# Layer 1 as seven unrolled tiles of 288 and 384 tokens, six chunks of weights to a pair of heads, turned probabilities in the place of the loaded v

## The reference

```
q, k, v: (4, 8, 576, 64)
q_d, k_d, v_d = means over 4 neighbouring tokens           # 144 tokens
out_up    = repeat(softmax_attention(q_d, k_d, v_d), 4)
scores    = q @ k.T / 8, masked to |i - j| < 4
out_local = softmax(scores) @ v
x = (out_up + out_local) as (2304 tokens, 512)
h = x @ w_in   (512 x 2048);  g = max(0.01 h, h);  x = g @ w_out  (2048 x 512)
h = x @ w_in2  (512 x 2048);  g = h - tanh(h);     out = g @ w_out2
```

## Time and profile before

| | |
|---|---|
| median of three runs | 953.19 us |
| the profiled execution | 953.53 us |
| its span, first to last instruction | 951.8 us |
| mean granted TensorE clock | 0.998 |
| busy: TensorE, VectorE, ScalarE, GpSimd | 939.1, 541.2, 557.2, 403.1 us |
| attention of the first batch | to about 43 us |
| layer 1 with attention between its chunks | about 44 to 432 us |
| layer 1 alone | about 432 to 537 us |
| layer 2 | about 537 us to the end |

### The profile page before, as it was taken

One profiled execution on the slowest core, in us unless ns is written; L12 is line 12 of the kernel. 1 busy time (PEld: TensorE's weight loads), 2 busy tenths in 40 slices (PEclk: granted clock), 3 DMA queues, 4 the chain that ended last, 5 costly groups with the idle time before them and its releaser, 6 DMA issues.

```text
span 951.8 us, 19930 instructions
## 1 busy us (share of the span) xinstructions
PE 939.1 (99%) x7026; PEld 882.9 (93%) x7026; DVE 541.2 (57%) x1078; ACT 557.2 (59%) x1351; POOL 403.1 (42%) x343
## 2 busy tenths in 40 slices
PE   8999999999999999999999999999999999999998
PEld 7799999999999999999999989899899898898997
DVE  6755445534544554453236576776666766766764
ACT  4665546445446455463446687666666756756754
POOL 3685417327246155171533667332233233233232
PEclk9999999999999999999999999999999999999999
DMA  7875111210121121102004022000000000000000
GB/s 159 192 197 141 46 33 27 51 36 26 39 51 26 25 51 40 38 2 67 1 2 134 12 58 86 30 5 1 34 0 0 33 0 0 33 0 0 34 1 33
DMA packets 87797, 41.48 MB, mean 44 GB/s; under 512 B 60352, under 2 KB 81344, under 8 KB 87744
## 3 DMA queue, kind: packets, MB, share of 16 engines
q1 hardware_dynamic: 87744, 40.78, 16.3%
HBM read 36.04 MB, written 4.72 MB: 43 GB/s over the span
## 4 chain that ended last, share of the span: by engine, by line
PE 88%; ACT 3%; POOL 3%; DVE 2%; DMA 2%; issue 1%; SPq 0%; ACTq 0%; DVEq 0%; POOLq 0%
PE ph L538 13%; PE ph L539 13%; PE ph L540 13%; PE acc L567 7%; PE acc L568 7%; PE acc L569 7%; PE acc L614 6%; PE acc L615 6%; PE acc L616 6%; PE banks L427 2%; PE banks L464 2%; PE banks L451 1%; POOL g_lo L1149 1%; PE banks L420 1%; POOL w_lo_b L1156 1%
## 5 line engine op out<-in xcount | busy, mean ns | idle before, releaser
L1149 POOL TENSOR_TENSOR g_lo<-scratch,g_hi 128x384 fp32r<-128x384 f32 x96 | 125.6, 1309 | 257.8 <-ACT g_hi L741 257.8
L996 DVE TENSOR_TENSOR ph<-g,ph 128x288 f32<-128x288 f32 x128 | 59.0, 461 | 165.4 <-ACT g L755 164.7
L538 PE MATMUL ph<-x_hi,w_hi_a 128*128 128x288 f32 (+1 forms) x448 | 143.6, 321 | 0.4 <-DVE x_lo L978 0.2
L540 PE MATMUL ph<-x_hi,w_lo_a 128*128 128x288 f32 (+1 forms) x448 | 139.9, 312 | 0.0
L539 PE MATMUL ph<-x_lo,w_hi_a 128*128 128x288 f32 (+1 forms) x448 | 139.9, 312 | 0.0
L1128 POOL TENSOR_TENSOR in_lo<-w_whole,in_hi 128x512 fp32r<-128x512 f32 x64 | 82.4, 1287 | 134.7 <-ACT in_hi L721 133.9
L755 ACT ACTIVATE g<-ph 128x288 f32<-128x288 f32 x128 | 52.5, 410 | 136.3 <-PE ph L540 136.3
L1133 POOL TENSOR_TENSOR out_lo<-w_whole,out_hi 128x512 fp32r<-128x512 f32 x64 | 86.0, 1343 | 71.8 <-ACT out_hi L725 71.6
L1030 DVE SCALAR_TENSOR_TENSOR scratch<-scratch,ph 128x384 f32<-128x384 f32 x96 | 53.2, 554 | 108.6 <-ACT scratch L804 104.0
L803 ACT ACTIVATE scratch<-ph 128x384 f32<-128x384 f32 x96 | 46.8, 487 | 108.4 <-PE ph L540 106.9
L983 DVE TENSOR_TENSOR g_lo<-ph,g_hi 128x288 fp32r<-128x288 f32 x128 | 58.6, 458 | 59.2 <-ACT g_hi L741 59.2
(11 more groups left out here) (273 smaller groups left out, 2660.4 us busy)
## 6 DMA issues: line engine op xcount, KB each, us to landing
out_dram<-o_stage SPq DMA_DIRECT2D x18, 256.0 KB, 2.1
w_whole<-in_moe_w_in_dram SPq DMA_DIRECT2D x16, 256.0 KB, 4.2
w_whole<-in_moe_w_out_dram SPq DMA_DIRECT2D x16, 256.0 KB, 4.9
qn<-in_q_dram SPq DMA_DIRECT2D x26, 144.0 KB
kn<-in_k_dram SPq DMA_DIRECT2D x26, 144.0 KB
v4n<-in_v_dram SPq DMA_DIRECT2D x26, 144.0 KB
vw<-in_v_dram SPq DMA_DIRECT2D x26, 122.5 KB
scratch<-in_moe_w_in_dram SPq DMA_DIRECT2D x8, 256.0 KB, 2.8
```

The lines of the kernel that those rows point to most:

```text
L538: pe.matmul(bank, whi, x_hi[:, c, 0:width], start=(c == 0), stop=False)
L540: last = pe.matmul(bank, wlo, x_hi[:, c, 0:width], start=False, stop=(c == CD - 1))
L996: dve.tensor_tensor(ph1[:, 1 - f % 2, 0:T1], g1[:, f % 2, :], ph1[:, 1 - f % 2, 0:T1], ALU.max)\
L1149: pool.tensor_tensor(g2_lo[:, f % 3, :], g2[:, f % 2, :], g2_hi[:, f % 3, :].bitcast(F32), ALU.subtract).then_inc(g_lo_done, 1)
```

## The change

- Layer 1 is cut into seven tiles of 288, 288, 384, 384, 384, 288 and 288 tokens, written out one by one (no loops) on every engine. Buffers of x, g and their halves grow to 384 columns.
- The twelve later pairs take 5 + 11 x 6 = 71 chunks of the 112, in place of 96 of 128. A plan gives for each engine and each of the six chunks two lists of steps: a first half, ahead of `down1` on TensorE, ahead of `split_in` and g_hi on ScalarE, ahead of g_lo on VectorE; and a second half, where the steps stood. The first pair (two steps of which are done earlier) takes five chunks.
- `v4n` and `pT` of buffer set A share one place; ScalarE's step 11 gets a wait for `vd_done`.

```diff
-GROUPS = ((0, 1), (2, 3), (4, 5), (6, 7, 8), (9, 10), (11, 12), (13, 14), (15, 16))
-GROUP_HEAD = 1
+SIZES = (288, 288, 384, 384, 384, 288, 288)
+NONE = ((), ())
+IN_SIX = {
+    "pe": (((0, 1), (2, 3)), ((), (4,)), ((), (6,)), ((), (11, 12)), ((), (13, 14)), ((), (15, 16))),
+    "act": (((0, 1), (2, 3)), NONE, ((7,), (8,)), ((), (11, 12)), ((), (13, 14)), ((), (15,))),
+    "dve": (((), (3,)), ((), (4, 5)), ((8,), (7,)), ((9,), ()), NONE, ((), (15, 16))),
+    "pool": (NONE, ((), (5,)), ((), (9,)), ((), (10,)), NONE, NONE),
+}
+IN_FIVE = {
+    "pe": IN_SIX["pe"][:4] + (((13, 14), (15, 16)),),
+    "act": IN_SIX["act"][:4] + (((13, 14), (15,)),),
+    "dve": IN_SIX["dve"][:4] + (((), (15, 16)),),
+    "pool": IN_SIX["pool"][:4] + (NONE,),
+}
+PLAN = (IN_FIVE,) + (IN_SIX,) * 11
...
-            A = PairBuffers("a", lambda name, shape: sb(name, shape, at=first), banks)
+            v4n_and_pT = sb("v4n_and_pT", [P, NB * P], at=first)
+            def place_a(name, shape):
+                if name in ("v4n", "pT"):
+                    return shaped(v4n_and_pT[0:shape[0], 0:math.prod(shape[1:])], shape)
+                return sb(name, shape, at=first)
+            A = PairBuffers("a", place_a, banks)
...
-        def later(f, tile, last):
-            if f < last:
-                pair, group = divmod(f + GROUP_HEAD, len(GROUPS))
-                for step in GROUPS[group]:
-                    yield step, A, 2 * tile + 1 + pair
+        def later(engine, tile, f, half):
+            at = CF * tile + f
+            for pair in range(len(PLAN)):
+                if f < CF and BEGINS[pair] <= at < BEGINS[pair + 1]:
+                    for step in PLAN[pair][engine][at - BEGINS[pair]][half]:
+                        if pair > 0 or step >= HEAD:
+                            yield step, A, pair + 1
...
-            with sp.Fori(1, MIXED) as tile:
-                for par in range(2):
-                    load_qk(A, 2 * tile + 1 + par, 4 * tile + 8 + 2 * par)
-                    load_v(A, 2 * tile + 1 + par, 4 * tile + 8 + 2 * par)
+            for i in range(3, len(PLAN) + 1):
+                load_qk(A, i, 2 * i + 6)
+                load_v(A, i, 2 * i + 6)
...
-            def layer1(tile, last, begun=True, ahead=True):
+            def layer1(tile, ahead):
                 for f in range(CF + LAG1):
-                    if f < CF and not (begun and f == 0):
+                    if 0 < f < CF:
                         hidden1(tile, f)
+                    for step, s, i in later("pe", tile, f, 0):
+                        attention(step, s, i)
                     if ahead and f == CF + LAG1 - 1:
                         hidden1(tile + 1, 0)
                     if f >= LAG1:
                         down1(tile, f - LAG1)
-                    for step, s, i in later(f, tile, last):
+                    for step, s, i in later("pe", tile, f, 1):
                         attention(step, s, i)
...
                 elif step == 11:
+                    act.wait_ge(s.vd_done, i + 1)
                     act.wait_ge(s.bank_full[1], uses1(i, 4))
...
+            def layer1(tile):                              # ScalarE
+                width, last = SIZES[tile], tile == TILES1 - 1
                 for f in range(CF + 1):
...
+                    if f == 0 and tile > 0:
+                        keep_y(tile - 1)
+                    for step, s, i in later("act", tile, f, 0):
+                        attention(step, s, i)
                     if KEPT <= f + 2 < CF:
                         split_in(tile, f + 2)
...
+                    if f == CF - 1 and not last:
+                        next_x(tile + 1)
+                    for step, s, i in later("act", tile, f, 1):
                         attention(step, s, i)
```

More of the change, by code:

```diff
@@ L85, in two_scale_attention_and_feed_forward, with columns1, pairs_below @@
     WHOLE = CF - KEPT
-    assert D == QB and DM == CD * P and LP * RUN == S and NB * QB == S and PAIRS == 4 + 2 * MIXED
+    assert D == QB and DM == CD * P and LP * RUN == S and NB * QB == S and PAIRS == 4 + len(PLAN)
+    assert sum(SIZES) == TOKENS
+    STARTS = [sum(SIZES[:tile]) for tile in range(TILES1)]
+    BEGINS = [sum(len(plan["pe"]) for plan in PLAN[:pair]) for pair in range(len(PLAN) + 1)]
+    def columns1(tile):
+        return slice(STARTS[tile], STARTS[tile] + SIZES[tile])
+    def pairs_below(tile):
+        return CD * ((STARTS[tile] + SIZES[tile] - 1) // S)
+    for tile in range(1, TILES1):
+        assert BEGINS[pairs_below(tile)] <= CF * tile - 1
     qv = q.rearrange("b h (p r) d -> p (b h) r d", r=RUN)
@@ L649, in _ @@
                 pe.wait_ge(s.bank_free[1], uses1(1, 0))
-            layer1(0, CF)
-            with pe.Fori(1, MIXED - 1) as tile:
-                layer1(tile, CF)
-            layer1(MIXED - 1, CF - GROUP_HEAD)
-            for tile in range(MIXED, TILES1):
-                layer1(tile, 0, ahead=tile < TILES1 - 1)
+            for tile in range(TILES1):
+                layer1(tile, ahead=tile < TILES1 - 1)
             layer2(0, begun=False)
@@ L868, in _ @@
             split_kept(EARLY)
-            mixed(0, nothing)
-            with act.Fori(1, MIXED - 1) as tile:
-                mixed(tile, lambda: keep_y(tile - 1))
-            mixed(MIXED - 1, lambda: keep_y(MIXED - 2), CF - GROUP_HEAD)
-            for tile in range(MIXED, TILES1):
-                last = tile == TILES1 - 1
-                layer1(tile, 0, w2a if last else nothing, lambda: keep_y(tile - 1),
-                       nothing if last else lambda: next_x(tile + 1))
-            split_x(x2_hi, T2, 0, N1)
+            for tile in range(TILES1):
+                layer1(tile)
+            split_x(x2_hi, T2, slice(0, T2), N1)
             keep_y(TILES1 - 1)
@@ L1074, in _ @@
             lo_of_first_x(CD - 1)
-            mixed(0, nothing)
-            with dve.Fori(1, MIXED - 1) as tile:
-                mixed(tile, lambda: keep_y(tile - 1))
-            mixed(MIXED - 1, lambda: keep_y(MIXED - 2), CF - GROUP_HEAD)
-            for tile in range(MIXED, TILES1):
-                last = tile == TILES1 - 1
-                layer1(tile, 0, w2a if last else nothing, lambda: keep_y(tile - 1),
-                       nothing if last else lambda: next_x(tile + 1))
-            lo_of_x(x2_hi, x2_lo, T2, 0, CD * TILES1)
+            for tile in range(TILES1):
+                layer1(tile)
+            lo_of_x(x2_hi, x2_lo, T2, slice(0, T2), CD * TILES1)
             keep_y(TILES1 - 1)
@@ L1139, in layer1 @@
                         split_in(tile, f + 2)
-                    for step, s, i in later(f, tile, last):
+                    for step, s, i in later("pool", tile, f, 1):
                         attention(step, s, i)
-                    if isinstance(tile, int) and tile == 0 and f + 3 < KEPT:
+                    if tile == 0 and f + 3 < KEPT:
                         split_kept(f + 3)
```

117 lines of the change are left out of this document (53 added, 64 removed).

## The result

The kernel after takes 958.93 us, the median of four runs (957.2 to 960.2), beside 953.06 for the kernel before: a ratio of 1.0057, with a 95% interval of 1.0045 to 1.0069. Its profiled execution took 957.17 us. It is slower by some 0.6%.

A forecast was written before the change was run, and what follows sets the result against it. TensorE's stream of matmuls plus its rare waits was taken as the bound. From the profiled 953.5 us, - 3.2 (gain) + 7.85 (waits) = 958.15; the median, 0.3 lower, 957.8 us, range 950.5 to 962.

The forecast's parts named there:

- part 1: Layer 1's wider tiles: 1152 matmuls of 384 columns replace 1536 of 288, a gain of 3.2 us (1.6 to 5.0).
- Part 2: Loops written out, loads of v, the shared place of `v4n` and `pT`, ScalarE's new wait: no cost.
- Pair 1: First later pair, five chunks during the kept weights' split: waits at steps 11 to 13, 4.0 us against 0.44, 3.6 net.
- Pairs 4 and 12: Pairs beginning at f = 1, no `down1` between steps 0, 1 and 2, 3: 0.9 us in all.
- Pairs 7 to 11: Later pairs at 384 columns, where a chunk gives the chain more time: they pay nothing.
- Pairs 2, 3 and 5: Pairs at 288 columns with weight splits, waits at steps 12 and 13: 0.35, 0.8 and 0.8 us.
- Pair 6: Third chunk at f = 15, fifth at f = 1: 1.4 us, 0.2 to 0.5 for x_lo, the rest at step 13.
- The sign to look for: TensorE's waits for probabilities and q, k turns (L451, L456): 6 to 8 us, 4 of them between 58 and 65 us.
- Faster, the chain keeps ahead: Steps 11 to 13 at 288 columns: waits of only 1 to 2 us, 949 to 951.3 us; chance 0.22.
- Near no change: Gain at its upper end, 5.0, against waits of 3 to 6 us: 951.3 to 955 us; chance 0.25.
- The delays pass on: Late leak delays g_lo and in_lo, each of twelve pairs pays 1 us: above 960, to 966 us; chance 0.13.
- the change doesn't do what it says: A 384-column matmul costs 4/3 of a 288-column one (0.177), so no gain; counted inside the forecast, no separate chance.

The follow-up runs named there:

- eight_wide: eight_groups with buffers of x, g and their halves 384 columns wide, tiles of 288 as before: 950.74 us, 0.9966 of before.
- eight_groups: The kernel after with the old eight tiles of 288 and old eight groups, loops still written out: 954.42 us, 1.0004 of before.
- kept_later: The kernel after with the splits of kept chunks 5 and 6 moved behind the attention steps of chunk 3: 955.85 us, 1.0026 of before.
- all288: The kernel after with eight tiles of 288 tokens and 288-column buffers, six-chunk plan kept: 967.16 us, 1.0147 of before.
- out_first: The kernel after with ScalarE splitting the out weights ahead of the next x at f = 15: 958.51 us, 1.0047 of before.
- two_orders: The kernel after with kept chunks 5 to 7 split later, and ScalarE's out_hi behind the next x but ahead of the steps: 951.17 us, 0.9975 of before.
- four_orders: three_orders with GpSimd also doing out_lo ahead of its attention steps at f = 15: 949.61 us, 0.9945 of before.
- after_again: The kernel after, unchanged, timed again as the measure for the others: 957.62 us, 1.0036 of before.
- three_orders: two_orders with VectorE's first half of steps at f = 15 moved behind x_lo: 952.86 us, 0.9990 of before.

## Why the prediction was right, and where it wasn't

The sign and the size were right: 957.8 us predicted, 958.9 and 957.6 measured. In the stretch -3.2 + 7.85 = +4.65 was predicted, -5.6 + 9.7 = +4.1 measured. But both terms were too small, and parts of the second were wrong in opposite ways: that the total came so near is luck, while the mechanism (TensorE comes too early to what the other engines hold back) is right.

- **The gain (part 1)** was put at 3.2 out of 1.6 to 5.0, and is 5.6. Two terms. The step at 384 is 173.8 ns, the better half of layer 2's chunk; I took the middle between the two halves for want of a reason, where the slow half comes right behind matmuls of 512 columns, which layer 1 doesn't have. That gives 1536 x 132.94 - 1152 x 173.8 = 4.0. The other 1.6 I had no term for: 1512 steps of 288 columns became 1.1 ns shorter because the buffers grew to 384 columns. eight_wide shows the shorter step with the width alone changed; what it brings in time is rather less than steps times 1.1 ns (2.4 us for 3.4 there).
- **Part 2** at nothing: right within 1 us, by eight_groups (0.7 us gained by writing out, 1.8 lost to one late load). The loads of v under the plan of six chunks aren't tested by it. In after GpSimd waited for them four times, 36.7 us in all; one wait, at the start, before has too (8.1 us), and in the chunks behind the other three (126.51, 211.44, 374.69) no row of TensorE shows a wait for GpSimd.
- **Pair 1** was put at 4.0 us (0.8, 0.5 and 2.7), 3.6 net. Measured, term by term: 0.62 of idle time ahead of step 11, some 0.3 ahead of step 12 for the exponentials, and 2.47 ahead of step 13: 3.4, of which 0.44 was there before, so some 3 net. The mechanism was that of the text, GpSimd's low part ahead of step 10, and kept_later took the wait away by moving that alone.
- **Pairs 4 and 12** at 0.9: 0.39 and 0.47. Right.
- **Pairs 7 to 11** at nothing: right, and all288 shows why: at 288 columns some of them wait.
- **Pairs 2, 3 and 5** at 0.35 + 0.8 + 0.8: measured 0, 0 and 0.31. This step failed. I let 0.4 us at step 12 stand as lost, at the end of a long sum of durations. In pair 3 the exponentials ended at 110.72, 3.63 us after `hidden1` began (107.09) and not 4.0; step 12 was reached at 110.78 and didn't wait. The sum had the maxima 0.35 us too late. (The 0.80 for L944 in the earlier trace rows, which the prediction held up as undisturbed, was taken with GpSimd idle and says nothing of contention; but at 56.10 in before the same sum ran beside GpSimd's low half and took 0.80 too.)
- **Pair 6** at 1.4: measured 0.77 for x_lo, nothing at step 13, 2.58 for out_lo and 1.6 by the clock, 5 us. This is the step that failed most. x_lo was put at 2.1 us of VectorE and took 2.91, for GpSimd's scaling beside it. I had x_lo ahead of VectorE's step 7, and followed that to `hidden1(0)` and to step 13 of the pair, but not to what else stands behind the same steps: out_hi in ScalarE's queue, behind exponentials that wait for step 7. I wrote out ScalarE's order in the front part, and then walked only the pair's own chain. out_first took this wait away, and two_orders, with x_hi in its place, made a gain of it; so the cause is shown.
- **Other turns** at nothing: 0.18 and 0.41 for out_lo, 0.27 for g_lo. By the last of them TensorE did wait for g_lo, which the prediction named as a sign against itself. It isn't the piling up that this sign was meant for: it is one wait, at 446.73, in a tile without attention.
- **The clock** wasn't foreseen. The prediction read the earlier trace rows as the full level throughout; but a 9 stands for 90% or more of a slice of 24 us. In before the granted clock was at 1.2 GHz from about 26.4 to 29.8 us, in the first batch:

```profile
26.00:30.00 4.00, 3.92 (x50) 3.29 (x49) 3.33 (x9) 0.80 (x2) 3.40 (x4) 0.57 0.81 212
```

The prediction said that there was nothing to win there, and didn't ask what a wait of over 2 us could lose there.

- **The sign to look for** was 6 to 8 us of waits at steps 11 to 14. They came to 3.4 of idle time and the 0.3 inside the group. More than half of TensorE's waiting was for out_lo, x_lo and the copy of q.

The idle times, 8.5 - 0.44 = 8.0, are near the 7.85 predicted because 1.6 too much for pairs 2, 3 and 5 and 0.9 too much for pair 1's idle time stood against 2.0 too little at pair 6 and 0.9 at the other turns. With the clock's 1.6 and the 0.3 inside a group they come to 9.9, beside 9.7 in the stretch.

**The rivals.** "Faster, the chain keeps ahead" needed GpSimd to do step 10 ahead of the kept part; the order in the queue forbade it, and two_orders, where it does, is faster than before. "Near no change" had the gain at its upper end, 5.0, near the 5.6 measured, but waits of only 3 to 6 us. "The delays pass on" isn't seen in after. That the change doesn't do what it says falls with the 384 step.

**What of the gain is the change's own.** four_orders is 949.61 us, and eight_wide, one number changed in the old plan, 950.74, with 498.07 and 499.41 in the stretch. So seven tiles and six chunks with mended orders are worth some 1.3 us in the stretch beyond what the wider buffers alone bring; as times, their ratios to before (0.9924 to 0.9966 and 0.9953 to 0.9979) overlap. Seven tiles have 112 chunks and the old groups need 95; seven tiles with the old eight groups weren't tried, and may keep the 4.0 us of the wider steps without most of the waits. That is open.

## What to carry to other kernels

When a step is moved so that it waits, list what stands behind it in each queue, and for each of those who waits for it: here one dear wait was for an attention step behind a weight split, the other for a weight split behind attention steps, and mending one queue passed the fault to the next until all three were in order. Ask too what the other engines will then do at the same time: out_lo, once it came early, slowed x_lo. When a change alters a buffer's width as a side effect, time that width by itself; it gave nearly as much here with one number (950.74 us) as the whole mended plan did (949.61). Compare stretches from a point behind the waits that differ: a late load made the width look worth 4.2 us in place of 2.4. A gain and a loss that nearly cancel should be checked apart, since a right total says little of its terms.

## What the runs showed of the hardware

- A matmul with 288 moving columns took 132.9 ns from start to start when the rows of its operand's buffer were 1152 bytes apart, and 131.8 to 131.9 at 1280 and 1536 bytes. Over the 3048 matmuls of the stretch the kernels part by 2.4 us. Why isn't known; where the buffers begin differed as well.
- After TensorE had idled 2.58 us, its granted clock fell to the 1.2 GHz level for about 3.4 us in after, and for some 6.8 in kept_later with the same wait (a mean of 0.65 over 190 to 195 and of 0.67 over 195 to 200 us). In after_again, and in all288 with its wait of 2.78, it fell as in after (0.66 over 195 to 200). In the kernels without this wait (out_first, two_orders, four_orders) it stayed at 1.00 there. In three_orders a wait of 1.98 us was not followed by a fall. In kept_later the fall began at 191.5, inside the wait, 0.7 us before its end. The length of the wait alone doesn't decide: in the first batch the clock fell at 18.7 us in after, behind a wait of 1.73 that ended at 17.05, and at 26.4 in before, behind one of 1.79 that ended at 24.54, while one of 1.85 in four_orders (to 17.36) had no fall.
- The same four subtractions of VectorE took 1.96, 2.91 and 4.00 us in three orders of the work: with no operation of GpSimd beside them, with one, and with two. The one or two that met it took 1.5 to 1.6 us each, the others some 0.5.
